# Small VectorE operations in other forms, and Pool's pooling held until both normalisations of a pair are done

## What is computed

```python
q_d, k_d, v_d = (x.reshape(B, H, Sd, 4, D).mean(axis=3) for x in (q, k, v))
out_up = np.repeat(sm_attn(q_d, k_d, v_d), 4, axis=2)       # attention over 144 pooled positions
mask = np.abs(pos[:, None] - pos[None, :]) < 4
attn = softmax(where(mask, scale * q @ k.T, -1e9))          # attention in a band of 7
x = out_up + attn @ v                                       # softmax divides by (sum + 1e-9)
h = x @ w_in0;  g = np.where(h > 0, h, np.exp(np.minimum(h, 0)) - 1);  x = g @ w_out0
h = x @ w_in1;  g = s * np.maximum(h, 0) ** 2 + b;                     out = g @ w_out1
```

## Time and profile before

| | |
|---|---|
| median of 3 runs | 944.8 us (942.14 to 945.2) |
| the profiled execution | 941.66 us |
| its span from first to last instruction | 939.9 us |
| mean granted clock of PE | 0.987 |
| busy: PE, DVE, ACT, Pool | 907.2, 417.0, 414.2, 153.5 us |

### The profile page before, as it was taken

One profiled execution on the slowest core, in us unless ns is written; L12 is line 12 of the kernel. 1 busy time (PEld: TensorE's weight loads), 2 busy tenths in 40 slices (PEclk: granted clock), 3 DMA queues, 4 the chain that ended last, 5 costly groups with the idle time before them and its releaser, 6 DMA issues.

```text
span 939.9 us, 16145 instructions
## 1 busy us (share of the span) xinstructions
PE 907.2 (97%) x5936; PEld 852.3 (91%) x5936; DVE 417.0 (44%) x773; ACT 414.2 (44%) x1104; POOL 153.5 (16%) x148
## 2 busy tenths in 40 slices
PE   6888789999999999999999999999999999999998
PEld 5767679999999999999999989989999899899996
DVE  6999964333233233233233353443443443443433
ACT  7988877534334344344366532232232232232222
POOL 6665627500000000000056500000000000000000
PEclk9998999999999999999999999999999999999999
DMA  8999715300000000000044300000000000000000
GB/s 199 195 198 181 144 46 146 101 1 1 1 1 0 0 0 0 0 1 1 1 123 125 90 1 1 34 1 1 34 0 0 34 0 0 34 1 0 35 1 34
DMA packets 42929, 41.47 MB, mean 44 GB/s; under 512 B 3616, under 2 KB 30080, under 8 KB 42880
## 3 DMA queue, kind: packets, MB, share of 16 engines
q1 hardware_dynamic: 42880, 40.83, 18.3%
HBM read 36.09 MB, written 4.72 MB: 43 GB/s over the span
## 4 chain that ended last, share of the span: by engine, by line
PE 86%; DVE 7%; issue 3%; SPq 2%; ACT 1%; DMA 1%; DVEq 0%; ACTq 0%
PE ps_h L513 43%; PE ps_y L534 21%; PE ps_y L532 21%; DVE stat L717 2%; DVE xy L777 1%; DVE prob L694 1%; DVE kd L687 1%; DMA wstage<-in_w_in 1%; DVE stat L707 1%; SPq L243 1%; DVE prob L728 1%; DVE stat L719 0%; PE ps_t L446 0%; SPq L239 0%; SPq L255 0%
## 5 line engine op out<-in xcount | busy, mean ns | idle before, releaser
L656 ACT ACTIVATE g_hi<-tmp 128x384 fp32r<-128x384 f32 x192 | 101.0, 526 | 262.4 <-PE ps_y L534 153.1
L797 DVE TENSOR_TENSOR g_lo<-tmp,g_hi 128x384 fp32r<-128x384 f32 x192 | 107.3, 559 | 205.2 <-ACT g_hi L656 205.2
L650 ACT ACTIVATE tmp<-ps_h 128x384 f32<-128x384 f32 x192 | 94.3, 491 | 227.1 <-PE ps_h L513 224.7
L513 PE MATMUL ps_h<-xs_hi,win_late_lo 128*128 128x384 f32 x576 | 193.8, 336 | 0.0
L513 PE MATMUL ps_h<-xs_hi,win_late_hi 128*128 128x384 f32 x576 | 193.8, 336 | 0.0
L513 PE MATMUL ps_h<-xs_lo,win_late_hi 128*128 128x384 f32 x576 | 193.6, 336 | 0.0
L789 DVE SCALAR_TENSOR_TENSOR tmp<-tmp,ps_h 128x384 f32<-128x384 f32 x96 | 53.2, 554 | 162.1 <-ACT tmp L653 161.2
L513 PEld LDWEIGHTS ps_h<-xs_lo,win_late_hi 128*128 128x128 f32 x576 | 108.3, 188 | 3.3
L513 PEld LDWEIGHTS ps_h<-xs_hi,win_late_hi 128*128 128x128 f32 x576 | 108.2, 188 | 3.2
L793 DVE TENSOR_TENSOR tmp<-tmp 128x384 f32<-128x384 f32 x96 | 55.2, 575 | 121.1 <-ACT tmp L650 121.1
L513 PEld LDWEIGHTS ps_h<-xs_hi,win_late_lo 128*128 128x128 f32 x576 | 108.3, 188 | 0.0
(11 more groups left out here) (86 smaller groups left out, 1457.8 us busy)
## 6 DMA issues: line engine op xcount, KB each, us to landing
wstage<-in_w_in SPq DMA_DIRECT2D x32, 256.0 KB, 2.7
wstage<-in_w_out SPq DMA_DIRECT2D x32, 256.0 KB, 2.8
kall<-in_kt SPq DMA_DIRECT2D x16, 288.0 KB, 5.9
qbd<-in_qt SPq DMA_DIRECT2D x32, 144.0 KB, 5.4
v<-in_v SPq DMA_DIRECT2D x16, 288.0 KB
out<-wstage SPq DMA_DIRECT2D x18, 256.0 KB, 2.2
vwin<-in_v SPq DMA_DIRECT2D x16, 224.0 KB
vwin<-in_v SPq DMA_DIRECT2D x32, 32.0 KB
```

Source lines behind the costliest of these rows:

```text
L513: mm = pe.matmul(o, w_chunk(0, a, j)[:, c * P:(c + 1) * P], xs[x][:, slot, c, :], start=(c == 0 and p == 0), stop=(c == CH - 1 and p == 2))
L650: act.activation(x, ps_h[:, j % 4, 0:TB], ACT.Relu, scale=-1.0 if layer == 0 else 1.0).then_inc(relu_ready, 1)
L656: act.activation(g[0][:, j % 2, :], x, ACT.Copy).then_inc(hi_ready, 1)
L797: dve.tensor_tensor(g[1][:, j % 2, :], x, g[0][:, j % 2, :].bitcast(F32), ALU.subtract).then_inc(g_ready, 1)
```

## The change

Three small things on DVE and one on Pool. On DVE, `max_pooled` writes its three maxima behind the pooled scores in PSUM and the scaling reads them there; `divisors` no longer adds 1e-9 with a scalar operation but sums planes 0 and 2 of `stat` with a reduction, plane 0 being filled with 1e-9 by one more memset at the start. On Pool, pooling of q runs one pair further ahead (pair 2 before the loop, pair i+3 in step i), and each step first waits until DVE has normalised both parts of pair i+1 (`probs_ready` 2i+4). The lines behind the edits move by 4 to 7 in the changed kernel: L711 becomes L717, L717 becomes L724, L728 L735, L736 L743, L777 L784.

```diff
@@ Pool
             pool_v(0, 0)
             pool.wait_ge(slots_zero, 2 * (CH - 1))
+            pool.wait_ge(dscores_ready, 1)
+            pool_q(0, 2)
 
             def step(n, u, left):
                 i = n * CH + u
-                if left >= 2:
-                    pool.wait_ge(dscores_ready, i + 1)
-                    pool_q(n + (u + 2) // CH, (u + 2) % CH)
+                if left >= 1:
+                    pool.wait_ge(probs_ready, 2 * i + 4)
+                if left >= 3:
+                    pool.wait_ge(dscores_ready, i + 2)
+                    pool_q(n + (u + 3) // CH, (u + 3) % CH)
                 if left >= 1:
                     pool.wait_ge(values_ready, i + 1)
                     pool_v(n + (u + 1) // CH, (u + 1) % CH)
@@ DVE
             dve.memset(stat[:], 1.0).then_inc(dve_order, 1)
+            dve.wait_ge(dve_order, 1)
+            dve.memset(stat[:, :, 0, :], 1e-9).then_inc(dve_order, 1)
...
-                dve.tensor_reduce(stat[0:2 * QD, u % 2, 0, NT:NT + NM],
+                dve.tensor_reduce(ps_sd[0:2 * QD, NM * SD:NM * SD + NM],
                                   ps_sd[0:2 * QD, 0:NM * SD].rearrange("p (m w) -> p m w", w=SD),
                                   AX_X, ALU.max).then_inc(max_ready, 1)
                 dve.wait_ge(max_ready, i + 1)
-                dve.tensor_scalar(stat[0:2 * QD, u % 2, 1, NT:NT + NM], stat[0:2 * QD, u % 2, 0, NT:NT + NM],
+                dve.tensor_scalar(stat[0:2 * QD, u % 2, 1, NT:NT + NM], ps_sd[0:2 * QD, NM * SD:NM * SD + NM],
                                   -SCALE / POOL ** 2, None, ALU.mult).then_inc(negmax_ready, 1)
...
-                dve.tensor_scalar(x, stat[0:rows, u % 2, 2, a:z], 1e-9, None, ALU.add).then_inc(recip_ready, 1)
+                sums = stat[0:rows, u % 2, 0:3:2, a:z].rearrange("p k t -> p t k")
+                dve.tensor_reduce(x, sums, AX_X, ALU.add).then_inc(recip_ready, 1)
```

More of the change, by code:

```diff
@@ L743, in split_x @@
                                   xs[0][:, slot, c, :].bitcast(F32), ALU.subtract).then_inc(x_split, 1)
-            dve.wait_ge(dve_order, 1)
+            dve.wait_ge(dve_order, 2)
             pool_k(0, 0)
```

## The result

The changed kernel takes 928.76 us (median of 4 runs, 928.61 to 932.17) against 943.71 (4 runs, 942.14 to 945.2): a ratio of 0.984, with a 95% interval of 0.981 to 0.987. The forecast was 928, range 921 to 937. The profiled execution is the slowest of the four, 932.17 with a span of 930.4; it is 9.5 us shorter than the profiled one of before, while the other three are 13 us shorter. So its steps are to be read with care: it shows the mechanisms, but at a lower mean clock of PE than its three companions (granted clock 0.986 against 0.991).

A forecast was written before the change was run, and what follows sets the result against it. DVE, standing for Pool's instructions, was taken to bound the attention stage. 15.8 (steps) + 1.0 (head) - 2.0 (loads) - 0.1 (tail) = 14.7 us off 941.66 gives 927.0; 1 added for the median: 928, range 921 to 937.

The forecast's parts named there:

- What bounds the kernel: Attention stage: DVE sets the pace, standing about 2.0 us a step for Pool, 26 us over 13 steps; feed-forward follows.
- The small operations: DVE's three small instructions a step no longer stand; the new forms cost 0.1 us a step, bounds 0 and 0.5.
- Rival 2: DVE's new small forms stand as the old ones: 13 steps lose 8 us, 936; chance 0.10.
- That the forms alone would pass much of the wait on: On DVE, a small operation that no longer stands passes much of its wait to its successor, so the hold is needed.
- The hold's timetable: Pool ends q and v at N+3.98, lo_w at N+5.36; L728, at N+4.3, stands 1.1 us with lo_w: step 7.05.
- Steps without lo_w at 6.25: Attention steps without lo_w: ACT sets 6.25 us (DVE would do 5.94), in 7 of the 13 steps.
- paid once: PE's or ACT's small wait for the pooled v at N+3.98 is paid once, unless the whole loop exceeds a step.
- rival 1: PE pauses over 1.2 us before L475 for pooled v, its clock falls: steps of 8.5 us, 951 or 954; chance 0.04.
- The sign that PE's clock in the attention would be nearer to 1.00: In the changed kernel's profile, PE's clock in the attention stage is nearer to 1.00; no size of change given.
- The head and the tail: Ahead of 23.06 two pairs gain 1.0 us (0 to 2.0); pair 15's later pool_v costs 0.1 us at the end.
- The loads: Late q landings make Pool, and with it PE, stand now and then: 2.0 us lost, bounds 0 and 4.
- Rival 3: ACT, PE, SP or DMA queues take gain: 7.0 to 7.2 us a step instead of 6.6, 933 to 936; chance 0.16.

The follow-up runs named there:

- almost no pooling: The kernel before with Pool's poolings of q and v cut to 8 columns each, lo_w whole: 930.2 us, ratio 0.987.
- the weights early: The changed kernel with the first weight blocks loaded 4 us earlier, before SP's loop: 934.1 us, ratio 0.990.
- The load experiments: Changed kernel, pool_v before pool_q, first weight blocks 4 us earlier; from batch 1 without v4's load: 924.8 us, or without three small window-row DMAs: 931.4 us.
- fewer bytes: Changed kernel, pool_v before pool_q, first weight blocks 4 us earlier, load of v4 (288 of 1179 KB a pair) left out from batch 1: 924.8 us, ratio 0.981.
- maxima's form alone: The kernel before with only max_pooled's two lines changed, maxima written to PSUM and scaling read there: 942.1 us, ratio 0.998.
- v first: The changed kernel with pool_v ahead of pool_q in each Pool step: 928.3 us, ratio 0.984.

## Why the prediction was right, and where its steps were not

What bounds the kernel: right. DVE set the pace of the attention and stood for Pool's instructions; with the standing gone, the stage is shorter and the feed-forward part follows as a block (PE's first feed-forward matmul starts at 124.07 instead of 133.55, 9.5 us earlier, and the span is 9.5 us shorter).

The small operations: right. I took 0.1 us a step between bounds of 0 and 0.5; the rows after show less than 0.02 in all (L713 +10 ns, L717 -8, L724 about the same as L717 before). The Trainium skill, VectorE: DVE Perf Modes, section "The TRN2 errata", has 120 cycles for a PSUM source where it has 58 for SBUF. This difference does not show at this size: 157 ns from PSUM, 165 from SBUF. Rival 2 is out. The prediction's memset of 96 elements is one of 24 and costs 78 ns, not 0.2 us.

That the forms alone would pass much of the wait on: wrong. They alone brought 13 us, and from a twenty-fifth to a fifth of a wait is passed on, not most. The forecast of the sum did not rest on it, since the hold was there too, but the reason I gave for needing the hold did: with the forms in, the medians put the hold at 2.4 or 3.9 us more (931.2 against 928.8 and 927.3, intervals that overlap), not half of the gain.

The hold's timetable: right to 0.2 us. Pool through q and v at N+3.98, lo_w then meeting L728 at N+4.3, a step of 7.05: the profile has N at 44.72, lo_w at N+4.1, L735 at N+4.15, and the three steps in which L735 stands for 1.1 us take 6.96 to 6.98. The other three of the six steps with lo_w take 6.95, 6.96 and 7.82 with less standing or none, so their mean of 7.10 agrees with the 7.05 partly by chance.

Steps without lo_w at 6.25: the term that was mis-sized. In the changed kernel's profile the seven of them take 7.32, 8.80, 7.02, 7.03, 6.17, 5.88 and 5.83 us, 6.86 in the mean. The 6.25 was meant as ACT's pace, and three steps lie below it; with almost no pooling ACT's steps take 5.87 without a weight copy, so the mean of 6.24 there matches the 6.25 only because every second step has a copy.

Two things were left out of the term. The larger one in this profile is the head of the stage: the steps of 7.32 and 8.80 lose 3.6 us against the forecast behind ACT's wait for the first weight block and PE's low clock after it. In the change measured again, and with the weights early, ACT has no such wait there, and one early step of 8.2 us stands behind a pause of 0.96 us for the pooled v and the low clock instead; so the two causes stand in for each other. The kernel before has such a step too (29.41 to 38.10, 8.69 us, with PE at its low clock), so not all that a step took above 5.84 was standing: measured against their shortest durations, DVE's five groups stood for 28 us over 16 pairs, 1.75 a pair where I took 2.0. The other is the pooled v: I let PE's wait for it be "paid once". It is paid again in 7 steps, 6.5 us in all, pauses of 0.67 to 1.29 us, because PE is faster than the step and catches up each time. After four of them (0.91, 0.93, 1.13, 1.29) the clock fell, after three (0.67, 0.76, 0.83) it did not. In the steps of 7.02, 7.03 and 7.82 this costs 0.8 us each against the forecast, 2.3 in all; the remaining steps are 1.3 us shorter than forecast.

That is rival 1's mechanism at its place, and it did not make the kernel slower. Its point of decision, a pause of over 1.2 us, does not hold even in the kernel before:

```profile
33.92 0.72 PE L475 MATMUL ps_xd<-probdt,vd 72*64 72x144 f32 x8 [0.92 <-ACT probdt L618]
...
36.92 1.59 PE L446 MATMUL ps_t<-ident,prob 128*70 128x128 f32 x8
...
67.62 1.06 PE L446 MATMUL ps_t<-ident,prob 128*70 128x128 f32 x8 [1.48 <-DVE prob L728]
```

After 0.92 us the next turning is slow, after 1.48 it is not. The 13 steps gained 11.2 us in the profile, not 15.8. The other three runs are about 3.5 us shorter in total, which the profile can't divide. The sign that PE's clock in the attention would be nearer to 1.00 did not come true (0.89 against 0.91 before, from 20 to 120 us).

The head and the tail: the head gained 1.5 us (1.0 forecast). The tail lost 3.2 (0.1 forecast): the steps to pair 14 and 15 take 7.63 and 4.36 us where they took 5.36 and 3.44, with PE at its low clock (its turning at 113.22 and 119.22 takes 2.2 us), behind one more pause of 1.13 us for the pooled v and one of 0.92 for ACT's copy.

The loads: right in kind. I took 2 us between 0 and 4 for landings that come late. The load experiments show them as the limit of the variants behind the change: at 6.3 us a step the bytes are too many, and ACT, or Pool, stands for them. In the changed kernel itself they are nearly in time in the first profile (Pool waits 1.6 us for q and 1.2 for v, ACT 1.5 for the first weight block) and late in the second one (Pool 9.2 us for q, ACT 4.6 for weight blocks). Rival 3, other engines taking part of the gain, is thus part of what happened, at the size of the terms above.

Sum: that 928 forecast and 928.8 measured agree so well is partly luck; the terms agree less. The profiled execution gained 9.5 us against 14.7 forecast for it, 4.6 of the difference in the 13 steps and 3.1 in the tail, less 2.0 allowed for loads and 0.5 of the head; but it lies 3.4 us above the median of its own kernel, where that of before lay 2 to 3 below. The medians gained 15.0 us (943.71 less 928.76), where the forecast had 16.8 from its 944.8.

## What to carry to other kernels

When an instruction's duration varies and nothing in it does, take its shortest case as its price and look on the other engines for an instruction that ends when it ends. Removing one contention is worth only the distance to the next bound: here half of the change brought nearly all of the gain, and the second half was for an engine that no longer set the pace. And before holding an engine back, ask for each instruction behind the hold who is waiting for it: the order inside the hold (v before q) decided whether PE paused for it, though the next wait, for ACT, took most of its place.

## What the runs showed of the hardware

An operation of three elements that takes 0.16 us alone lasted up to 1.24 us while Pool's instruction was under way, when it was a scalar operation with its input in SBUF. Reductions (810 to 811 ns for L702), the reciprocal (215 or 216 ns on the mean for 9 elements in the profiles), the scaling that reads PSUM (156 to 157 ns), and the operations with one input in PSUM and one in SBUF (404 to 524 ns for L694 and L777) did not; this agrees with the Trainium skill, SBUF — State Buffer, section "Who interferes with whom", in which a reduction never contends and an operation with one SBUF input outside the two-port modes does not.

The time of one and the same changed kernel goes with the granted clock of PE: the runs with the new forms alone go from 925.8 us at a mean clock of 0.996 to 938.3 at 0.983, the seven of the change measured again from 925.5 at 0.996 to 935.0 at 0.983. The kernel before, in which DVE set the pace, does not show this so plainly: 11 runs beside the last experiments lie between 941.4 and 945.5 us at 0.982 to 0.989, in no order. The falls that were looked at came behind pauses of PE at a late wait, but the length of the last pause does not decide it. Falls followed 0.68 us (fewer bytes, at 46.98), 0.91, 0.92, 1.13 and more; none followed 1.20 (the change measured again, at 81.12), 1.48 (before, at 67.62) or 1.57 (maxima's form alone, at 72.91). What decides stays open. So does the question whether v first is worth anything: its profile lost the waits and its median lost nothing that can be told.

With the DMA share at 1.02 to 1.06 the loads of q, k, v and weights ran at 168 to 214 GB/s in stretches of 20 us. In such a stretch a weight block of 256 KB took 8.5 us to land, where it takes 2.7 on the median of the whole kernel.
